# Attention of a fused attention and two-MLP kernel: two score items to a step, and the inverse row sums by way of DRAM

## The reference

```python
# q, k, v: 4 x 8 heads x 576 tokens x 64
scores = (1 / 8) * q @ k.T
scores = where(pos_i // 64 >= pos_j // 64, scores, -1e9)   # block-causal mask
attn = exp(scores - max(scores))
attn = attn / (sum(attn) + 1e-9)
x = (attn @ v) arranged as 2304 tokens x 512
h = x @ w_in;  x = (h * tanh(softplus(h))) @ w_out          # 512 -> 2048 -> 512
xn = x / sqrt(mean(x * x) + 1e-6) * rms_g
out = (silu(xn @ w_gate) * (xn @ w_val)) @ w_out2           # 512 -> 1536 -> 512
```

## Time and profile before

| | |
|---|---|
| median of 3 runs | 1046.78 us (1045.84 to 1047.9) |
| profiled execution | 1047.26 us, span 1045.5 us |
| PE, PEld busy | 1012.5 us (97%), 923.2 us (88%) |
| DVE, ACT, POOL busy | 657.3 us (63%), 447.3 us (43%), 174.1 us (17%) |
| granted TensorE clock, mean | 0.995 |

### The profile page before, as it was taken

The page is one execution under the profiler, slowest core; times in us unless marked ns, Lnnn a source line. Parts: engine busy times, 40 slices in busy tenths (PEclk is TensorE's granted clock), DMA queues, the critical chain, the costliest instruction groups (busy, mean ns, idle before and its releaser), DMA issues.

```text
span 1045.5 us, 18028 instructions
## 1 busy us (share of the span) xinstructions
PE 1012.5 (97%) x6788; PEld 923.2 (88%) x6788; DVE 657.3 (63%) x1275; ACT 447.3 (43%) x964; POOL 174.1 (17%) x149
## 2 busy tenths in 40 slices
PE   6999999989999999999899799999999999999997
PEld 4666666689999999999898799999999999999996
DVE  4777777779999998999999975612323224124111
ACT  4555555545454554545455444522323123214212
POOL 3444446220000000000300130102130131031000
PEclk9999999999999999999999989999999999999999
DMA  7456555211010010100003125210020020100101
GB/s 164 122 135 160 151 132 132 67 54 31 1 62 1 31 31 2 60 0 34 27 13 90 55 66 172 61 61 1 1 61 1 3 61 1 59 3 1 31 1 31
DMA packets 96320, 56.67 MB, mean 54 GB/s; under 512 B 60144, under 2 KB 86768, under 8 KB 96240
## 3 DMA queue, kind: packets, MB, share of 16 engines
q1 hardware_dynamic: 96240, 55.59, 18.9%
HBM read 41.42 MB, written 14.16 MB: 53 GB/s over the span
## 4 chain that ended last, share of the span: by engine, by line
PE 88%; DVE 8%; issue 3%; ACT 1%; SPq 0%; DMA 0%; ACTq 0%; DVEq 0%
PE ps L1019 26%; PE ps L979 15%; PE ps L962 14%; PE ps L1037 13%; PE ps L928 4%; PE ps L921 4%; PE ps L915 4%; PE ps L903 2%; DVE elementwise L760 1%; DVE gHL L770 1%; PE ps L935 1%; DVE elementwise L763 1%; DVE elementwise L757 1%; PE ps L888 1%; PE ps L1083 1%
## 5 line engine op out<-in xcount | busy, mean ns | idle before, releaser
L962 PE MATMUL ps<-xHL,w_in_slots 128*128 128x384 f32 x1152 | 203.2, 326 | 1.4 <-DVE ms L783 0.7
L979 PE MATMUL ps<-gHL,w_early 128*128 128x384 f32 x1008 | 181.7, 331 | 14.7 <-DVE gHL L770 14.5
L962 PEld LDWEIGHTS ps<-xHL,w_in_slots 128*128 128x128 f32 x1152 | 189.5, 189 | 2.0 <-issue 2.0
L979 PEld LDWEIGHTS ps<-gHL,w_early 128*128 128x128 f32 x1008 | 167.6, 191 | 19.0 <-DVE gHL L770 15.0
L1019 PE MATMUL ps<-xHL,w_in_slots 128*128 128x384 f32 x864 | 151.3, 326 | 0.8 <-issue 0.8
L1019 PEld LDWEIGHTS ps<-xHL,w_in_slots 128*128 128x128 f32 x864 | 142.9, 189 | 2.7 <-issue 1.2
L851 DVE TENSOR_TENSOR ub<-ps,silu 128x384 f32<-128x384 f32 x72 | 40.1, 556 | 147.3 <-PE ps L1019 128.2
L605 ACT ACTIVATE uHL<-ub 128x384 fp32r<-128x384 f32 x72 | 37.7, 523 | 219.4 <-PE ps L1037 198.3
L854 DVE TENSOR_TENSOR uHL<-ub,uHL 128x384 fp32r<-128x384 f32 x72 | 50.9, 706 | 122.5 <-ACT uHL L605 122.5
L1019 PE MATMUL ps<-xHL,w_early 128*128 128x384 f32 x648 | 114.1, 326 | 0.0
L524 ACT ACTIVATE elementwise<-ps 128x384 f32<-128x384 f32 x96 | 47.0, 490 | 155.6 <-PE ps L962 146.2
(11 more groups left out here) (119 smaller groups left out, 1500.4 us busy)
## 6 DMA issues: line engine op xcount, KB each, us to landing
stage<-in_moe_w_out SPq DMA_DIRECT2D x28, 256.0 KB, 3.1
x_scratch<-xT SPq DMA_DIRECT2D x16, 288.0 KB, 2.2
xraw<-x_scratch SPq DMA_DIRECT2D x12, 384.0 KB, 4.1
x_scratch<-x2sb SPq DMA_DIRECT2D x6, 768.0 KB, 3.9
xraw<-x_scratch SPq DMA_DIRECT2D x6, 768.0 KB, 5.6
out_x<-osb SPq DMA_DIRECT2D x18, 256.0 KB, 3.0
raw_q<-in_q SPq DMA_DIRECT2D x32, 128.0 KB, 2.6
raw_k<-in_k SPq DMA_DIRECT2D x32, 128.0 KB, 2.5
```

The costliest lines, as they stand in the source:

```text
L962: mm = pe.matmul(ps[:, f % 4, 0:N], w[:, b, t], alternate(xHL[par][:, a, t]), start=n == 0, stop=n == 11, skip_group_check=True)
L979: mm = pe.matmul(ps[:, 4 + t, 0:N], slot_of(f)[:, b, t * P:(t + 1) * P], alternate(gHL[f % 4][:, a]), start=f == 0 and n == 0, stop=f == F ...
```

## The change

Step g is put in another order. PE makes the scores of items 0 and 1, then the values of tiles 3 and 2 of pair g-1, then the transposes in one row (tiles 1, 0 and 4 of g-1; tails, queries and keys of g+1), then the scores of items 2 and 3, then the values of tiles 1, 0 and 4 of g-1, then the transposes of tiles 3 and 2 of g. Eleven uses a step take the banks 4, 5 and 6 in turn (`ring`), so that each use waits for the copy of the one three before it. The inverse sums are written into the eight empty columns of the last tile's probabilities, are transposed along with them, are stored to DRAM by SP and loaded again, broadcast over 64 rows; DVE copies the products to `x_sum` and POOL multiplies.

```diff
+    r_dram = nc.dram_tensor("r_scratch", (8, P), F32, kind="Internal").ap()
-        rinv_wide = sb("rinv_wide", [P, 4, P], at=attn)
+        x_sum = sb("x_sum", [P, 512], at=attn)
-        TR = (4, 5, 6)
+        (PT1, PT0, PT4A, PT4B, QUERIES, KEYS, PV4, PT3A, PT3B, PT2A, PT2B), USES = range(11), 11
+        def ring(g, use):
+            return 4 + (USES * g + use) % 3
+        inverses = prob4[:, S:S + 8]
...
# SP
             def store_pair(g):
-                sp.wait_ge(xT_done, 2 * g + 2)
+                sp.wait_ge(xT_done, g + 1)
+                sp.wait_ge(x_last, g + 1)
                 sp.dma_start(x_dram[g], xT[:]).then_inc(x_stored, 16)
+            def store_inverses(g):
+                sp.wait_ge(pT_out, 8 * g + 8)
+                sp.dma_start(r_dram, pT4[64:72, 4]).then_inc(r_stored, 16)
+            def load_inverses(g):
+                sp.wait_ge(r_stored, 16 * (g + 1))
+                need(sp, xT_done, g)
+                for p in range(2):
+                    rows = r_dram.rearrange("(t h) (o q) -> h o t q", h=2, o=1)[p].broadcast_to([64, 4, P])
+                    sp.dma_start(rinv_all[64 * p:64 * p + 64].rearrange("p (t q) -> p t q", t=4), rows)\
+                        .then_inc(r_in, 16)
...
-            for g in range(PAIRS):
+            for g in range(PAIRS + 1):
                 if g + 2 < PAIRS:
                     load_qk(g + 2)
                 for u in (2 * g + 2, 2 * g + 3):
                     if u < 2 * F1:
                         load_unit(u)
+                if g >= 2:
+                    store_pair(g - 2)
                 if g >= 1:
-                    store_pair(g - 1)
+                    store_inverses(g - 1)
                     if g + 1 < PAIRS:
                         load_v(g + 1)
+                    load_inverses(g - 1)
...
# GpSimd: spread_inverse_sums is gone
+            def scale_x(g):
+                pool.wait_ge(r_in, 32 * (g + 1))
+                pool.wait_ge(x_summed, g + 1)
+                need(pool, x_stored, 16 * g)
+                pool.tensor_tensor(xT[:, 0:512], x_sum[:], rinv_all[:], ALU.mult).then_inc(xT_done, 1)
             for u in range(2 * F1):
-                if u % 2 == 0 and u >= 2:
-                    spread_inverse_sums(u // 2 - 1)
+                if u % 2 == 0 and u >= 6:
+                    scale_x(u // 2 - 3)
                 split_unit(u)
...
# ScalarE: inverse_sums_out is gone, keys_out stands right behind queries_out
                 exp_item(g, 0)
-                if g >= 1:
-                    inverse_sums_out(g - 1)
                 exp_item(g, 1)
                 if g + 1 < PAIRS:
                     queries_out(g + 1)
+                    keys_out(g + 1)
                 exp_item(g, 2)
-                if g + 1 < PAIRS:
-                    keys_out(g + 1)
                 exp_item(g, 3)
...
# VectorE
             def x_out(g):
                 dve.wait_ge(pv_done, 4 * g + 3)
-                dve.wait_ge(r_out, g + 1)
-                need(dve, x_stored, 16 * g)
-                dve.tensor_tensor(xT[:, 0:512], ps[:, PVB], rinv_all[:], ALU.mult).then_inc(xT_done, 1)
+                need(dve, xT_done, g)
+                dve.tensor_copy(x_sum[:], ps[:, PVB]).then_inc(x_summed, 1)
             def x_last_out(g):
                 dve.wait_ge(pv_done, 4 * g + 4)
-                dve.tensor_copy(xT[:, 512:S], ps[:, TR[2], 0:64]).then_inc(xT_done, 1)
+                need(dve, x_stored, 16 * g)
+                dve.tensor_copy(xT[:, 512:S], ps[:, ring(g + 1, PV4), 0:64]).then_inc(x_last, 1)
...
# VectorE's order in a step after: invert_sums(g-1), row_max 0, normalise_last(g-1), row_max 1,
#   probT_out of tiles 1, 0, 4, 4 of g-1, tails_out(g+1), row_max 2, row_max 3, x_last_out(g-1),
#   probT_out of tile 3 (two halves) and tile 2 (two halves) of g, x_out(g-1)
# TensorE, step g after
                 if cur:
                     scores(g, 0)
                     scores(g, 1)
                 if last:
                     need(pe, x_summed, g - 1)
                     pe.wait_ge(v_in[(g - 1) % 2], 48 * ((g - 1) // 2 + 1))
                     pe.wait_ge(pT_out, n + 4)
                     pv(g - 1, 3).then_inc(pv_done, 1)
                     pv(g - 1, 2).then_inc(pv_done, 1)
                     pe.wait_ge(exp_done, 4 * g - 1)
                     probT(g - 1, 1, 0, ring(g, PT1), 0)
                     probT(g - 1, 1, 1, ring(g, PT1), 256).then_inc(pT_ps, 1)
                     probT(g - 1, 0, 0, ring(g, PT0), 0)
                     probT(g - 1, 0, 1, ring(g, PT0), 128).then_inc(pT_ps, 1)
                     pe.wait_ge(norm_done, g)
                     for j in range(4):
                         tr = pe.transpose(ps[:, ring(g, PT4A), P * j:P * j + P], prob4[:, P * j:P * j + P], ident[:])
                     tr.then_inc(pT_ps, 1)
                     pe.wait_ge(pT_out, n + 5)
                     pe.transpose(ps[:, ring(g, PT4B), 0:P], prob4[:, 512:640], ident[:]).then_inc(pT_ps, 1)
                 if more:
                     pe.wait_ge(tail_out, g + 1)
                     tails(g + 1)
                     need(pe, pT_out, n + 6)
                     queries(g + 1)
                     need(pe, pT_out, n + 7)
                     keys(g + 1)
                 if not cur:
                     up(0, 0, 0, 0, True, False)
                 if cur:
                     scores(g, 2)
                     scores(g, 3)
                 if last:
                     pe.wait_ge(pT_out, n + 8)
                     pv(g - 1, 1)
                     pv(g - 1, 0).then_inc(pv_done, 1)
                     if more:
                         pe.wait_ge(tail_out, g + 2)
                     pv_last(g - 1)
                 if cur:
                     pe.wait_ge(exp_done, 4 * g + 2)
                     if more:
                         pe.wait_ge(q_out, g + 2)
                     probT(g, 3, 0, ring(g, PT3A), 0).then_inc(pT_ps, 1)
                     if more:
                         pe.wait_ge(k_out, g + 2)
                     probT(g, 3, 1, ring(g, PT3B), 0).then_inc(pT_ps, 1)
                     need(pe, x_last, g)
                     if more:
                         pe.wait_ge(tail_out, g + 2)
                     probT(g, 2, 0, ring(g, PT2A), 0).then_inc(pT_ps, 1)
                     pe.wait_ge(pT_out, n + 9)
                     probT(g, 2, 1, ring(g, PT2B), 0).then_inc(pT_ps, 1)
                 else:
                     up(1, 0, 1, 0, True, False)
```

More of the change, by code:

```diff
@@ L404, in _ @@
                         .then_inc(xL_done, 1)
+            for g in range(PAIRS - 3, PAIRS):
+                scale_x(g)
             def x_low(c, n, par):
@@ L735, in _ @@
                 if cur:
-                    row_max(g, 3)
-                    probT_out(g, 1, pT2[:, 0], TR[1], 0)
-                    probT_out(g, 1, pT2[:, 1], TR[2], 1)
+                    probT_out(g, 0, pT3[:, 0], ring(g, PT3A), 0)
+                    probT_out(g, 0, pT3[:, 1], ring(g, PT3B), 1)
+                    probT_out(g, 1, pT2[:, 0], ring(g, PT2A), 0)
+                    probT_out(g, 1, pT2[:, 1], ring(g, PT2B), 1)
+                if last:
+                    x_out(g - 1)
             def mish_numerator(s, f):
@@ L1089, in _ @@
                     tails(g + 1)
+                    need(pe, pT_out, n + 6)
+                    queries(g + 1)
+                    need(pe, pT_out, n + 7)
+                    keys(g + 1)
+                if not cur:
+                    up(0, 0, 0, 0, True, False)
+                if cur:
+                    scores(g, 2)
+                    scores(g, 3)
                 if last:
-                    if not cur:
-                        up(1, 0, 1, 0, True, False)
+                    pe.wait_ge(pT_out, n + 8)
@@ L1093, in _ @@
                     pv(g - 1, 1)
                     pv(g - 1, 0).then_inc(pv_done, 1)
-                if more:
-                    need(pe, r_out, g)
-                    queries(g + 1)
-                if cur:
-                    scores(g, 2)
-                    pe.wait_ge(exp_done, 4 * g + 1)
-                    need(pe, pT_out, 2 * (4 * g - 1) + 1)
-                    probT(g, 3, 0, TR[0], 0).then_inc(pT_ps, 1)
-                    need(pe, pT_out, 2 * (4 * g - 1) + 2)
                     if more:
@@ L1116, in _ @@
-                if more:
-                    pe.wait_ge(pT_out, 2 * (4 * g) + 1)
-                    keys(g + 1)
-                if cur:
-                    scores(g, 3)
-                    pe.wait_ge(exp_done, 4 * g + 2)
-                    pe.wait_ge(pT_out, 2 * (4 * g) + 2)
-                    probT(g, 2, 0, TR[1], 0).then_inc(pT_ps, 1)
-                    need(pe, xT_done, 2 * g)
-                    if more:
-                        pe.wait_ge(q_out, g + 2)
-                    probT(g, 2, 1, TR[2], 0).then_inc(pT_ps, 1)
-                    need(pe, xT_done, 2 * g - 1)
-                    pe.wait_ge(v_in[g % 2], 48 * (g // 2 + 1))
```

(13 more changed lines are left out.)

108 lines of the change are left out of this document (43 added, 65 removed).

## The result

The changed kernel takes 1050.21 us (median of 7 runs, 1048.11 to 1052.13) against 1047.01 us (7 runs) for the kernel before: ratio 1.0032, 95% interval 1.0019 to 1.0044, **3.2 us slower**. The prediction was 1042.3 us, range 1034 to 1049, with 0.18 for slower: wrong in direction, and the time lies outside the range.

What follows compares the result with a forecast made beforehand. A loop through DVE and PE, tied by the ring of three banks, was taken to bound attention's steps. Steps -4.3, start -1.9, end +0.8 and +0.9 gave -4.5: from 1046.78 to 1042.3 us, range 1034 to 1049.

Steps and rivals of the forecast that it cites:

- PE's own work: Attention step on PE: eight fewer shape changes and four fewer transposes cut its work from 12.84 to 11.05 us.
- The loop through DVE: Attention steps: DVE's part 7.78 plus PE's way back 4.75 makes 12.53 us against 12.84; 4.3 gained over 14 steps.
- PE's way back: From tile 4's first-half copy through keys, scores, values and transposes until DVE has tile 3's result: 4.75 us.
- The start: Step 0: item 3's scores need only item 1's exponentials, so step 1 starts at 19.4 instead of 21.36: 1.9 gained.
- The end: Last attention steps into the MLP: two losses, 0.8 us until DVE starts the MLP and 0.9 from a late up(1).
- First term: From step 15's start to DVE starting the MLP: 20.5 us against 19.7, 0.8 lost.
- Second term: MLP entry: up(1) and its exponential last until 12.2, where DVE wants it at 11.3: 0.9 lost.
- Bounds 0 and 0.19 a step; I take 0, nearer to the ordinary row.: POOL's new multiply overlapping normalise_last in SBUF: 0 to 0.19 us a step, 2.7 in all; taken as 0.
- The sums may be 3.3 us later.: Inverse sums' round trip by DRAM, before x_last_out: 3.3 us in hand; beyond that every us adds one a step.
- fourth rival: Inverse sums come late at x_last_out: slower, one for one beyond 3.3 us; 1 us beyond gives 1061; chance 0.10.
- Rival 5: PE's clock falls in attention between values and scores, from transposes and waits: +4 us a step, 1100 us; chance 0.05.
- The sum: Whole kernel: -4.3 - 1.9 + 0.8 + 0.9 = -4.5 us, so 1046.78 becomes 1042.3.

Runs made afterwards that it cites:

- j_norm_act: c_both plus x_out on ScalarE, up(0) first in the last step, two buffers for x's last columns, and normalise_last's multiply on ScalarE: 1034.8 us, ratio 0.9884.
- d_xout_act: c_both with x_out of pairs 0 to 14 on ScalarE instead of VectorE: 1039.27 us, ratio 0.9914.
- i_norm_act: c_both with the multiply of normalise_last on ScalarE, ahead of item 0's exponentials: 1037.08 us, ratio 0.9908.
- b_split: Changed kernel with POOL's split of the first x moved directly behind its multiply scale_x(10), ahead of unit 26's split: 1045.37 us, ratio 0.998.
- a_loadx: Changed kernel with the first load of x moved in SP's queue from round 7's end to round 8, behind store_inverses: 1046.97 us, ratio 0.9996.
- c_both: Changed kernel with both the first load of x and POOL's split of the first x moved: 1042.95 us, ratio 0.9962.
- h_no_trip: Changed kernel without the loads of the inverse sums, which are set to 1 once by GpSimd: 1045.2 us, ratio 0.9984.

## Why the prediction was wrong, step by step

- **PE's own work.** Right as far as it can be read: 15 changes of shape became seven, and eight of the holes of 0.17 are gone. Of the seven left three are 0.07 to 0.12, among them the boundary between items 2 and 3, and the three such of the kernel before were like that. j_norm_act comes within 0.8 of the 11.05, and its weight loads wait 0.80 a step for DVE's copies (0.26, 0.36 and 0.18 at 102.55, 107.97 and 108.90).
- **The loop through DVE.** Right in mechanism, too long by 0.28: 12.25 for 12.53. PE's way back is 4.77, where 4.75 was reckoned. DVE's part is 7.48 for 7.78: the inversion is 0.31 (95.86 to 96.17) for 0.39, row maxima 0 are 1.09 for 1.14, and the normalisation with its two small operations 0.82 (97.26 to 98.08) for 0.99. For the inversion the reason is plain: the 0.39 was counted to the end of the reciprocal, and the next operation starts 0.09 ahead of that end. For the other two the rows don't say why. That DVE and not PE set the pace is shown by d_xout_act and i_norm_act, where work taken from DVE shortens the step.
- **The start.** 1.6 gained, 1.9 predicted. The keys now stand ahead of item 2's scores, which therefore begin at 15.68 instead of 15.05, and item 3's scores at 16.66, where 16.2 was reckoned:

```profile
16.66 0.20 PEld L928 LDWEIGHTS ps<-kT,qT 64*64 64x64 f32 x4
```

The two operations of DVE that were held at 20.70 and 23.34, for 0.86 and 0.50 us, come behind the start and belong to step 1.
- **The end.** First term 0.63 for 0.8. Second term 1.30 for 0.9: `up(1)` was late as said.
- **"Bounds 0 and 0.19 a step; I take 0, nearer to the ordinary row."** This step failed. The price isn't a share of bandwidth. It is what is left of POOL's operation, up to 3.4 us, and it lay nowhere in the bound, since I priced only the multiply (1.27 us) and took the 0.19 from one row. The ordinary row that I leaned on, 0.52 with POOL at work too, is one in which DVE was 0.07 us ahead and POOL waited (102.03 and 102.10 above); it says nothing of the case in which POOL is first. POOL's 6.2 us on the first x, which the kernel before runs in a gap (168.9 to 175.2, where every operation of DVE has an operand in PSUM; it inverts its sums at 175.3), kept their place behind unit 25's split. What DVE does at that time was changed around them. Price: 6.0 us in step 12, 5.4 of it given back by b_split.
- **"The sums may be 3.3 us later."** This failed too. I followed the round trip through SP's queue in an ordinary step, with a store of x landing in 2.2 us. It lands in 3.4 now, for a reason that stays open, and in one round the load of x is in that queue ahead of the store. The wait it turns into is the fourth rival's, at the place named there (`x_last_out`), but once and not in every step: 3.0 us, 3.8 given back by a_loadx.
- **The clock.** Rival 5 had it fall in every step because of the many transposes. It did not: steps of 12.25 run at 1.00, with 21 transposes in a row. It fell behind the two stalls and made them dearer, by 1.2 us and up to 1.9.
- **The sum.** Ordinary steps would have given more than predicted. With both events moved away the same change takes 1042.95 us (c_both), where 1042.3 was predicted. That agreement is in part luck, as a faster loop and remaining held steps cancel.

Open: why single issues on SP take about 2 us (L276 at 109.51, 1.98 of the 2.53 above; h_no_trip has such ones too), why the store lands later, and PE's pause of 0.65 us in the second MLP.

## What to carry to other kernels

Before an engine's order is changed, look up for every operation of VectorE from SBUF to SBUF which GpSimd operation will run at that time, the long one-off ones above all. If GpSimd's starts first, the price of a meeting is the whole rest of it; if VectorE's starts first, GpSimd waits, so a shift of a tenth of a us can turn a free meeting into a dear one. Multiplies and additions over several columns met this here, reciprocals and reads of PSUM did not. Follow a new transfer through its queue also in the one round in which something else is issued, and reckon with a low clock behind a stall of TensorE: here stalls of 1.8 us and more had it.

## What the runs showed of the hardware

- VectorE's addition over 128x8 and its multiply over 128x576, source and destination in SBUF, wait until GpSimd's running operation has ended: 2.65 us for 128x8 elements, and 88 such ends of 88 lie 0.02 to 0.32 us behind GpSimd's. Reciprocals over 128x8 and 128x1 and additions over 128x1 don't (0.20, 0.16 and 0.14 us beside it).
- Where VectorE's multiply started 0.07 us ahead, GpSimd's addition took 1.34 us instead of 1.04.
- After PE pauses of 1.8 and 3.85 us the granted clock fell to 0.50 and stayed there for 3.4 and 6.8 us, while PE was busy again for most of it. A pause of 1.40 us (b_split, step 9) left it at 1.00.
- 21 transposes in a row a step, in 12.25 us, left it at 1.00 too.
- One transfer's issue took 1.98 us in SP's queue, where its neighbours took 0.5 to 0.8.
- ScalarE's multiply from SBUF to SBUF, in place of VectorE's, brought the steps from 12.25 to 11.87 and their outliers down (i_norm_act).
